# Attention of the first batch in units of two heads instead of one

## The reference

```python
scores = scale * np.matmul(q, k.transpose(0, 1, 3, 2))      # q, k, v: 2 batches, 8 heads, 768 tokens, 64
keep = is_sink | in_window                                  # 4 sinks, window of 128 tokens
scores = np.where(keep, scores, -1000000000.0)
a = np.exp(scores - np.max(scores, axis=-1, keepdims=True))
a = a / (np.sum(a, axis=-1, keepdims=True) + 1e-09)
x = np.matmul(a, v)                                         # then heads side by side: (2, 768, 512)
u = x + (x.transpose(0, 2, 1) @ U @ V).transpose(0, 2, 1)   # first mixer, rank 32
y = u + np.maximum(u @ w_ch1, 0.0) @ w_ch2                  # 512 -> 2048 -> 512
h = np.maximum(y.transpose(0, 2, 1) @ w_tok1, 0.0) @ w_tok2 # second mixer, 256 wide
u = y + h.transpose(0, 2, 1)
out = u + np.maximum(u @ w_ch1, 0.0) @ w_ch2                # 512 -> 1536 -> 512
```

## Time and profile before

| | |
|---|---|
| median of 3 runs | 636.92 us (636.3 to 639.7) |
| profiled execution | 637.81 us, its span 635.7 us |
| PE busy (matmul) | 617.1 us, 97% of the span |
| DVE, ACT, POOL busy | 357.9, 325.9, 399.3 us |
| attention of the first batch on PE | from about 9 us to about 77 us |

### The profile page before, as it was taken

The page is one execution under the profiler, slowest core; times in us unless marked ns, Lnnn a source line. Parts: engine busy times, 40 slices in busy tenths (PEclk is TensorE's granted clock), DMA queues, the critical chain, the costliest instruction groups (busy, mean ns, idle before and its releaser), DMA issues.

```text
span 635.7 us, 10351 instructions
## 1 busy us (share of the span) xinstructions
PE 617.1 (97%) x3466; PEld 556.7 (88%) x3466; DVE 357.9 (56%) x757; ACT 325.9 (51%) x728; POOL 399.3 (63%) x420
## 2 busy tenths in 40 slices
PE   7899889999999999999999999999999999999997
PEld 6788689999998988989999988899998888999986
DVE  6776754564554466685665741396577226665411
ACT  5657666555555555754454444545454447454321
POOL 8654557978878675566575654576656446667252
PEclk9999989999999999999999999999999999999999
DMA  8545343553342525322223342442323353421152
GB/s 171 107 100 118 84 98 101 124 128 102 100 117 82 153 79 152 83 84 83 100 84 110 90 107 75 120 113 83 97 88 114 93 144 96 148 84 34 51 153 78
DMA packets 88468, 65.59 MB, mean 103 GB/s; under 512 B 43041, under 2 KB 72481, under 8 KB 88417
## 3 DMA queue, kind: packets, MB, share of 16 engines
q1 hardware_dynamic: 88416, 64.95, 37.5%
HBM read 61.52 MB, written 3.15 MB: 102 GB/s over the span
## 4 chain that ended last, share of the span: by engine, by line
PE 85%; DVE 8%; issue 3%; ACT 2%; POOL 1%; DMA 1%; DVEq 0%; SPq 0%; ACTq 0%; POOLq 0%
PE bank L1584 32%; PE bank L1340 23%; PE bank L1549 10%; PE bank L1416 4%; PE bank L1386 3%; PE bank L1513 3%; PE bank L1463 3%; PE bank L1396 2%; PE bank L1363 1%; PE bank L1489 1%; DVE b_lo L1209 1%; DVE masked L1108 1%; PE bank L1444 1%; PE bank L1576 1%; DVE k_hi L1086 1%
## 5 line engine op out<-in xcount | busy, mean ns | idle before, releaser
L852 POOL TENSOR_TENSOR w_lo<-w_raw,w_hi 128x512 fp32r<-128x512 f32 (+1 forms) x158 | 211.5, 1345 | 137.6 <-ACT w_hi L873 137.1
L873 ACT ACTIVATE w_hi<-w_raw 128x512 fp32r<-128x512 f32 (+1 forms) x158 | 96.7, 618 | 53.5 <-PE bank L1584 35.5
L1584 PE MATMUL bank<-w_hi,hid_hi 128*128 128x512 f32 x216 | 86.6, 401 | 0.9 <-DVE hid_lo L1040 0.9
L1584 PE MATMUL bank<-w_hi,hid_lo 128*128 128x512 f32 x216 | 85.1, 394 | 0.0
L1584 PE MATMUL bank<-w_lo,hid_hi 128*128 128x512 f32 x216 | 84.8, 392 | 0.0
L923 ACT ACTIVATE probs<-masked,neg_max 128x264 f32<-128x264 f32 x96 | 49.5, 516 | 66.7 <-DVE neg_max L1108 65.9
L1584 PE MATMUL bank<-w_hi,y_hid 128*128 128x512 f32 x216 | 71.1, 394 | 0.2
L1108 DVE CUSTOM_DVE_ANT_0 masked<-bank,masks 128x264 f32<-128x264 f32 x96 | 41.1, 429 | 28.8 <-PE bank L1386 25.4
L1416 PE MATMUL bank<-v_nat,probs_T 128*128 128x64 f32 x352 | 50.4, 262 | 1.5 <-DVE probs_T L1127 1.2
L1416 PEld LDWEIGHTS bank<-v_nat,probs_T 128*128 128x128 f32 x352 | 48.0, 190 | 3.3 <-DVE probs_T L1127 1.6
L1584 PEld LDWEIGHTS bank<-w_hi,y_hid 128*128 128x128 f32 x216 | 40.6, 188 | 9.5 <-POOL w_lo L852 1.5
(11 more groups left out here) (175 smaller groups left out, 1502.3 us busy)
## 6 DMA issues: line engine op xcount, KB each, us to landing
w_raw<-in_moe_w_ch_dram SPq DMA_DIRECT2D x144, 256.0 KB, 2.7
w_raw<-in_moe_w_ch_dram SPq DMA_DIRECT2D x20, 512.0 KB, 3.5
q_nat<-in_q_dram SPq DMA_DIRECT2D x12, 256.0 KB, 3.3
k_nat<-in_k_dram SPq DMA_DIRECT2D x12, 256.0 KB, 4.1
v_nat<-in_v_dram SPq DMA_DIRECT2D x12, 256.0 KB, 4.4
out_dram<-o_stage SPq DMA_DIRECT2D x11, 256.0 KB, 3.3
w_raw<-in_moe_w_tok_dram SPq DMA_DIRECT2D x6, 256.0 KB, 2.7
w_raw<-in_moe_w_tok_dram SPq DMA_DIRECT2D x8, 192.0 KB, 2.3
```

Of the source, the lines that this page charges most:

```text
L852: nc.gpsimd.tensor_tensor(w_lo[:, split % NW, 0:n], w_raw[:, split % NR, 0:n], w_hi[:, split % NW, 0:n].bitcast(f32), ALU.subtract) \
L873: nc.scalar.activation(w_hi[:, split % NW, 0:n], w_raw[:, split % NR, 0:n], ACT.Copy) \
L1584: last = mm(m_tile(use)[:, :], stationary, w[:, slot, :], start=False, stop=(final and n == 2), skip_group_check=True)
```

## The change

From the second tile of the first batch on (u >= 8), two heads make one unit. Each kind of step is gathered over both heads: first the preparations of both, then both scores, both value products, both probability transposes, and `down` last. The second batch and the first tile keep their order. No instruction is added or dropped but one wait on POOL, after its own two selects of `triangles`.

```diff
@@ attention(b)
-            now += scores + turned + pv + probsT + sinks
-            if u == hi and b == 0:
-                now.append(("ksinks", NQ))
+            after = [("ksinks", NQ)] if u == hi and b == 0 else []
             if b == 0 and h == 5 and T > 0:
-                now.append(("down", 1, b, T - 1))
-            units.append(now)
+                after.append(("down", 1, b, T - 1))
+            if b or u < H or u % 2 == 0:
+                units.append([now, scores, turned, pv, probsT, sinks, after])
+            else:
+                for kind, more in zip(units[-1], (now, scores, turned, pv, probsT, sinks, after)):
+                    kind += more
+        units = [[s for kind in unit for s in kind] for unit in units]
         return units
@@ block.gpsimd, at the step ("pv", H)
                         nc.gpsimd.affine_select(out=part, in_=part, compare_op=ALU.is_ge, fill=0.0, base=-n,
                                                 pattern=[[step, P]], channel_multiplier=-step) \
                           .then_inc(triangles_built, 1)
+                    pool.wait_ge(triangles_built, 3)
```

## The result

The changed kernel takes 642.33 us (median of 5 runs, 642.21 to 644.97); the kernel before, in 5 runs beside it, 636.92 (636.3 to 639.7). The ratio is 1.0092, 95% interval 1.0065 to 1.0119: about 5.9 us slower. Forecast were 642.6 and case (a).

A forecast was written before the change was run, and what follows sets the result against it. PE bounds the kernel (85% of the last chain, busy 10.36 of 10.46 us a steady tile). Terms 0 + 1.5 + 1.5 + 0.5 + 1.2 + 1.0 = 5.7 us on the median 636.92 give 642.6, range 638.5 to 645.8.

The forecast's parts named there:

- case (a): The forecast itself: waits of about half a us at three places of each tile; chance 0.70, range 640.5 to 645.
- first grouped tile: Stretch 14.30 to 24.94: some idle time goes, new waits come; taken as 0, bounds -1.5 and +0.7 us.
- two steady tiles: Tiles starting at 24.94 and 35.40: three new waits of 0.50 us, so 1.5 us longer each.
- third tile, V's parts: Tile starting at 45.86: new waits 1.5, less 1.3 wait for V's parts, plus 0.3 remaining: 0.5 us.
- last tile: Last full tile: new waits 1.5, plus 0.42 for longer key casts, less 0.71 excess already there: 1.2 us.
- tail: Behind the last such `down` (D): last `sinkpv` at D + 7.4 instead of D + 6.36, 1.0 us later.
- The query and key transposes: Tiles 2 to 5, twice a tile: they wait for DVE's copy of the last even head, 0.50 us each (0.47 to 0.56).
- `down` and `x_nat`: Each tile's end: `down` waits longer for `x_nat` behind DVE's copy, casts and two maskings; 0.50 us more a tile.
- POOL's wait: New wait of POOL after its own selects: holds up only POOL, costs nothing.
- rival (d): PE's clock falls in the attention as behind 76.52 us; one such stretch more, 644.3; chance 0.06.
- Rival (b): DVE catches up during the two new waits, so `x_nat` doesn't come later; 2.6 us slower, 639.5; chance 0.19.
- Rival (c): New waits don't show; PE loses three quarters of its idle time ahead of the mixer, 4 us: 632.9; chance 0.05.

The follow-up runs named there:

- pair67: Against the kernel before: only heads 6 and 7 of each tile form one unit, all other heads keep their order; 639.46 us, ratio 1.0061.
- pair01: Against the kernel before: only heads 0 and 1 of each tile form one unit; 640.23 us, ratio 1.0055.
- pair45: Against the kernel before: only heads 4 and 5 of each tile form one unit; 638.92 us, ratio 1.0030.
- pair23: Against the kernel before: only heads 2 and 3 of each tile form one unit; 640.08 us, ratio 1.0044.
- turn_first_early: Changed kernel with a pair's probability transposes ahead of its value products and `sinkpv` with `x_nat` first in the unit of heads 4 and 5; 642.86 us, ratio 1.0086.
- early: Kernel before with `sinkpv`, reciprocal and `x_nat` moved ahead of the key casts and head 4's masking; 635.51 us, ratio 0.9980.
- early_v: Kernel before with `sinkpv` and `x_nat` first in head 4's unit, and V's parts made at query transposes of tiles 5 and 6; 633.86 us, ratio 0.9951.
- pairs_early: Changed kernel with `sinkpv` and `x_nat` first in the unit of heads 4 and 5, ahead of key casts and both maskings; 640.28 us, ratio 1.0060.
- turn_first: Changed kernel with both probability transposes of a pair ahead of both its value products; 646.65 us, ratio 1.0149.

## Why the prediction was right, point by point

Measured is the growth of the distance between starts of `down`; the sum is that of the prediction.

| term | predicted | measured |
|---|---|---|
| first grouped tile | 0 | +0.15 |
| two steady tiles | 1.5 + 1.5 | 1.53 + 1.55 |
| third tile, V's parts | 0.5 | 0.59 |
| last tile | 1.2 | 1.39 |
| tail | 1.0 | 0.56 |
| sum | 5.7 | 5.77 |

**The query and key transposes** were mis-sized downwards: 0.50 taken, 0.56 measured, at the upper end of its bounds (0.47 to 0.56). DVE's copy started 0.43 behind the transposes and took 0.42, as in the earlier trace rows, and PE went on 0.15 behind it, as in the row 79.79 of the earlier trace rows, not 0.06 as ahead of `down`. pair67 and pair01 show each of the two alone.

**`down` and `x_nat`** were mis-sized upwards: +0.50 taken, +0.33 measured (0.64 instead of 0.31). From head 0's transposes it took 3.33 (45.76 to 49.09), where 3.43 was worked out: I let the casts follow at the end of the copy, 0.42 after its start, but DVE started them after 0.34 (46.18 to 46.52). And `down` was due at +2.69, not +2.64. The allowance for the sinks' subtraction, which took the estimate up, wasn't needed. pair45 confirms the size, 0.34 and 0.36. The two errors, +0.12 and -0.17, nearly cancel. The three waits make 0.56 + 0.56 + 0.33 = 1.45 of the 1.53 and 1.55; the last 0.1, a few hundredths in each group of two, is put down to nothing here. That the steady tile came out at 1.54 is in part luck.

**V's parts.** The value product of head 34 waited 0.6 before; after the change the row is

```profile
51.00 1.10 PE L1420 MATMUL bank<-v_nat,probs_T 128*128 128x64 f32 x8
```

It starts 1.91 behind `down`. In the tile before, with the same two scores between and no wait, it was 1.66 (37.08 to 38.74), so 0.25 is waiting, and the eight take 1.10 instead of 1.00, another 0.1: 0.35 is left, where 0.3 was forecast. The sum 1.54 - 1.30 + 0.35 gives the measured 0.59. Inside the term two sizes were off and cancelled: from V's first cast to the product it is 2.05 (48.95 to 51.00) and not 2.21, since that cast took 0.55 instead of 0.72 (not explained here), and `down` with two scores covers 1.66 and not 1.79. The scores of heads 6 and 7 alone don't do it: pair67 has them too, and there PE waited for ACT's copy instead.

**Last tile.** +1.39 against 1.2, but not for the reason given. The forecast carried the long key casts of before (1.27 instead of 0.85) over, and with them a longer wait of `down`:

```profile
70.12 0.79 PE L1400 MATMUL bank<-ident,probs 128*128 128x128 f32 x4
71.43 0.85 DVE L1090 CAST k_hi<-uT_full 64x512 fp32r<-64x512 f32 x2
71.72 1.22 PE L1420 MATMUL bank<-v_nat,probs_T 128*128 128x64 f32 x8
```

The casts took 0.85 here. `down` was due at 72.78 + 0.44 = 73.22 and started at 74.00: it waited 0.78, and before 0.87 (67.70 + 0.22 to 68.79). So `down` gave 0.1 back instead of costing the 0.2 that the sum of 1.2 left for it. What made up for it are two delays that the sum did not have: from head 0's transposes to the next score it is 0.54 (70.12 to 70.66) instead of 0.36, and from the value products to the next transposes 1.06 (71.72 to 72.78) instead of 0.84. (These come to 1.43 with the two waits of 0.56; a product that was 0.1 late before and the 0.1 that is open in each tile cancel.) DVE was late ahead of both: two casts for the queries (68.19) took 1.84 where they had taken 0.86 (63.32), with POOL busy on two instructions from 68.25 on, and the sinks' subtraction came only at 70.07. The step that failed is "the key casts take 1.27 instead of 0.85, 0.42 on the way to `x_nat`"; that the term is right to 0.2 is luck.

**Tail.** The one term whose size is clearly off: 1.0 forecast, 0.56 measured. With D = 74.00, DVE, ACT's sinks and PE:

```profile
77.40 1.10 PE L1420 MATMUL bank<-v_nat,probs_T 128*128 128x64 f32 x8 [0.30 <-DVE probs_T L1131]
78.34 0.60 PE L1400 MATMUL bank<-ident,probs 128*128 128x128 f32 x4
78.77 0.42 DVE L1131 COPY probs_T<-bank 128x256 f32<-128x256 f32 x1 [1.42 <-PE bank L1400]
79.51 0.44 DVE L1102 TENSOR_TENSOR k_lo<-uT_full,k_hi 64x48 fp32r<-64x48 f32 x2
80.60 0.28 DVE L1135 TENSOR_TENSOR p_sinkT<-bank,p_sinkT 32x128 fp32r<-32x128 f32 x1 [0.65 <-ACT p_sinkT L945]
80.94 0.50 PE L1429 MATMUL bank<-v_sink,p_sinkT 96*128 96x512 f32 x1
```

The steps on PE came as worked out: head 44's product at D + 3.40 (3.5), head 46 at D + 4.34 (4.3), its copy at D + 4.77 (4.7). But the last `sinkpv` stood 2.17 behind the copy, not 2.65: I had carried the distance of the earlier trace rows over, and in it DVE's `k_lo` took 1.54. Here it took 0.44, and what `sinkpv` then waited for is the chain of the sinks through ACT, which the prediction didn't follow. The step that failed is "the last `sinkpv` 2.65 later".

**First tile, POOL's wait, clock.** The first grouped tile moved by 0.15, inside its bounds, as gains and losses nearly cancel: idle times of 0.37 and 0.78 ahead of probability transposes (for ACT's copies) are gone, and there are new ones of 0.42 (a score, for POOL's `k_lo`) and 0.46 (the key transposes), while `down` sits idle for 0.70 instead of 0.40. PE is busy for 8.56 of 10.15 us there from the first stalled value product on. No wait is put down to POOL's new one. The granted clock was 1.00 in every stretch of the first batch's attention, in all eleven kernels, so rival (d) did not happen, although PE stood still three times in 12 us. The Trainium skill (TensorE: Matmul & The Clock Gate, A second HAM failure mode: psum-queue depth-cycling) says that small idles between groups of matmuls that cycle through PSUM banks made the clock oscillate in another kernel, one of bf16 matmuls; no run here shows a fall of the clock within the first batch's attention.

**Rival (b)**, DVE catching up during the new waits, is refuted by the same rows: the copy, casts, maskings and `x_nat` follow one another from 46.18 to 48.35 with no gap, so DVE's spare time elsewhere in the tile is no use to `down`. **Rival (c)** needed the copy to be out after 0.44; it was out after 0.85.

**From the profile to the median.** 5.7 was put on the difference of the whole; the ratio gives 5.9, the medians 5.4, the last `down` 5.77. The prediction said that nothing later gives the loss back, and without the fall of the clock that holds: from the last `down` to the end it is 557.9 us after the change and 557.8 or 557.9 in the six other kernels without a fall (last section). It said nothing of the mixer's clock, by which the two spans differ by 4.5 only.

## What to carry to other kernels

Where an engine issues in order and two buffers alternate, ask of every pair of writes to one buffer how much work lies between them: here one unit of 0.98 us covered a copy that is out 0.85 us after its transposes begin, and grouping by two left 0.44. Where such a wait is the same in every tile, look first at the order of the other engine: here two edits that moved DVE's work brought PE to no recorded idle time in three tiles, and regrouping PE's own work only added to it. Distrust durations that are carried over from the old trace: the two that were, 1.27 and 1.54 us, took 0.85 and 0.44 in the new order. And try each part alone as well as together: the waits didn't add, because one hid behind another.

## What the runs showed of the hardware that was not expected

**The clock behind the attention fell in four of eleven profiled executions.** Over 72 to 96 us the granted clock averaged 0.93 before, in pair23 and in turn_first_early, 0.86 in pair45, and 1.00 in the seven others. The two long idle times of PE there are alike in all of them (1.5 us ahead of query transposes, 1.4 ahead of the mixer's first matmul). What it costs shows between the start of the last `down` and the end of the span: 557.8 to 557.9 us in the seven executions without a fall, 559.0 to 559.2 in the three with 0.93, 559.9 in pair45. So the fall is worth 1.1 to 2.0 us, up to a third of the effect that was to be measured, and two spans alone would have been 1.3 us off. Each kernel was profiled once, but the timed executions of a single kernel differ in the same way: early took 634.3 to 635.5 us in five executions with a mean clock of 1.000 and 636.2 to 636.5 in three with 0.995. Which executions get the fall was not found. Before, in the stretch of 6 us that holds those matmuls:

```profile
82.00:88.00 6.00, 4.93 (x22) 4.80 (x23) 3.09 (x8) 2.79 (x8) 2.47 (x3) 0.72 0.17 44
```

**Two DVE instructions took 1.54 or 0.44 us.** The subtractions for `k_lo` (64x48) behind the last even copy took 1.53 or 1.54 in all in five kernels (before, pair45, pair23, early, early_v), and in each of them POOL's 1.27 us instruction on `w_lo` had started 0.02 or 0.03 ahead of them (73.22 and 73.25 before, 74.10 and 74.12 in pair45). They took 0.43 or 0.44 in the six others (after, pair67, pair01, pairs_early, turn_first, turn_first_early), where no such instruction of POOL ran beside them. In the kernel before POOL's ends at 73.22 + 1.27 = 74.49 and DVE's at 74.79, 0.30 later: as if DVE had stood until POOL was through. The Trainium skill (SBUF — State Buffer, SBUF: two separate sides) says so: a DVE instruction with two inputs from SBUF and a GpSimd instruction that reads SBUF share a port pair that whichever starts first keeps to its end. All eleven executions agree with it; no kernel here was made to test it. For the forecast it means that a moved DVE instruction is not worth its old duration.
